# Down projections of an MoE kernel: each pass of a contraction chunk goes to both token tiles in turn

## What is computed

```python
for e in range(E):                       # 8 experts, D = 512, F = 1024
    mask = expert_idx == e
    h = np.maximum(x[mask] @ w1[e], 0.0)
    out[mask] = gate_w[mask, None] * (h @ w2[e])
...
h = np.maximum(x @ w_in, 0.0)            # 512 -> 2048
return (h * h @ w_out).astype(np.float32)    # 2048 -> 512
```

## Time and profile before

| what | value |
|---|---|
| median of 3 runs | 599.38 us |
| the three runs | 595.86, 599.38, 601.61 us |
| span of the profiled execution | 599.6 us |
| its mean granted TensorE clock | 0.980 |
| expert stage, first up matmul to the end of the last down | 139.0 to 307.6 us |
| feed-forward, first up matmul to the end | 319.1 to 599.6 us |

### The profile page before, as it was taken

The page is one execution under the profiler, slowest core; times in us unless marked ns, Lnnn a source line. Parts: engine busy times, 40 slices in busy tenths (PEclk is TensorE's granted clock), DMA queues, the critical chain, the costliest instruction groups (busy, mean ns, idle before and its releaser), DMA issues.

```text
span 599.6 us, 11061 instructions
## 1 busy us (share of the span) xinstructions
PE 578.1 (96%) x4259; PEld 506.3 (84%) x4259; DVE 285.5 (48%) x422; ACT 251.2 (42%) x517; POOL 95.7 (16%) x125
## 2 busy tenths in 40 slices
PE   7898999999999999999999999999999999999997
PEld 6776776599899898898888989889899998988986
DVE  5989886565556465475563223223323323222321
ACT  4788886824445544354452123222222212222221
POOL 7467850031022021130210000000000000000000
PEclk9789889989999999999999999999999999999999
DMA  7967896058676494684711002002001001000000
GB/s 223 262 201 209 227 188 181 27 176 303 233 272 224 149 317 134 226 281 147 271 62 44 1 1 72 0 1 70 0 0 70 0 0 69 1 0 36 1 0 36
DMA packets 66044, 70.68 MB, mean 118 GB/s; under 512 B 25784, under 2 KB 50360, under 8 KB 65632
## 3 DMA queue, kind: packets, MB, share of 16 engines
q1 hardware_dynamic: 62400, 58.17, 32.0%
q0 software_dynamic: 3616, 12.13, 5.8%
HBM read 60.22 MB, written 10.06 MB: 117 GB/s over the span
## 4 chain that ended last, share of the span: by engine, by line
PE 63%; issue 12%; DMA 11%; POOL 6%; DVE 4%; ACT 1%; SPq 1%; POOLq 1%; ACTq 0%; DVEq 0%
PE psum L799 19%; PE psum L801 19%; PE psum L800 19%; DMA x_rows_sb<-x_rows,idx_g 5%; DMA win_raw<-in_moe_w_in 3%; PE psum L592 3%; POOL win_lo L495 2%; DVE wa_lo L1340 2%; PE psum L793 1%; POOL win_hi L493 1%; DMA v_blk<-in_v 1%; ACT wa_hi L1019 1%; POOL v_blk L506 1%; PE psum L852 1%; DMA q_raw<-in_q 1%
## 5 line engine op out<-in xcount | busy, mean ns | idle before, releaser
L799 PE MATMUL psum<-x_hi,win_hi 128*128 128x256 f32 x384 | 108.4, 282 | 1.2 <-DVE x_lo L1388 1.2
L801 PE MATMUL psum<-x_hi,win_lo 128*128 128x256 f32 x384 | 108.4, 282 | 0.0
L800 PE MATMUL psum<-x_lo,win_hi 128*128 128x256 f32 x384 | 108.2, 282 | 0.0
L1398 DVE TENSOR_TENSOR h_sq<-h_relu 128x512 f32<-128x512 f32 x48 | 33.3, 694 | 133.4 <-ACT h_relu L1073 133.4
L1073 ACT ACTIVATE h_relu<-psum 128x512 f32<-128x512 f32 x48 | 28.7, 599 | 134.6 <-PE psum L801 134.6
L799 PE MATMUL psum<-wb_hi,h_hi 128*128 128x512 f32 x208 | 83.4, 401 | 0.0
L800 PE MATMUL psum<-wb_lo,h_hi 128*128 128x512 f32 x208 | 82.3, 396 | 0.0
L801 PE MATMUL psum<-wb_hi,h_lo 128*128 128x512 f32 x208 | 82.2, 395 | 0.0
L799 PEld LDWEIGHTS psum<-x_hi,win_hi 128*128 128x128 f32 x384 | 73.3, 191 | 2.9 <-issue 1.4
L800 PEld LDWEIGHTS psum<-x_lo,win_hi 128*128 128x128 f32 x384 | 73.3, 191 | 1.7
L801 PEld LDWEIGHTS psum<-x_hi,win_lo 128*128 128x128 f32 x384 | 73.3, 191 | 0.0
(11 more groups left out here) (184 smaller groups left out, 998.0 us busy)
## 6 DMA issues: line engine op xcount, KB each, us to landing
w_raw<-in_moe_w SPq DMA_DIRECT2D x56, 512.0 KB, 3.9
win_raw<-in_moe_w_in POOLq DMA_DIRECT2D x8, 512.0 KB, 5.8
w_raw<-in_moe_w_out SPq DMA_DIRECT2D x8, 512.0 KB, 4.0
k_raw<-in_k SPq DMA_DIRECT2D x8, 384.0 KB, 5.1
q_raw<-in_q SPq DMA_DIRECT2D x8, 384.0 KB, 5.0
v_blk<-in_v SPq DMA_DIRECT2D x3, 1024.0 KB, 6.0
v_win<-in_v SPq DMA_DIRECT2D x16, 192.0 KB
x_rows<-x_all SPq DMA_DIRECT2D x8, 384.0 KB, 4.7
```

What stands on the lines that cost most here:

```text
L799: pe.matmul(o, l_hi, r_hi, start=start, stop=False)
L800: pe.matmul(o, l_hi, r_lo, start=False, stop=False)
L801: return pe.matmul(o, l_lo, r_hi, start=False, stop=stop)
L1398: dve.tensor_tensor(h_sq[c % 2][:, :], h_relu[c % 2][:, :], h_relu[c % 2][:, :], ALU.mult)\
```

## The change

A new helper `three_both` issues the three passes of a product for both token tiles in turn: high by high for tile 0, then for tile 1, high by low for tile 0, then 1, low by high for tile 0, then 1. Successive matmuls so write the two banks of `ps_y` alternately, and the two of a pair have the same moving operand. In the feed-forward the sequence inside a chunk is all that changes. In `expert_down` the loop over token tiles goes inside the loop over chunks: both tiles are now summed over all 8 chunks together, both waits for the previous block's copies out of PSUM stand ahead, and `y_summed` gets its two increments from the last two matmuls of the whole down projection. What waits for `y_summed` on ACT and DVE is as it was. Thirteen empty lines at the top of the file also go, so that line numbers are 13 lower ahead of the new helper.

```diff
+            def three_both(l_hi, l_lo, r_hi, r_lo, start, stop):
+
+                for t in range(2):
+                    pe.matmul(ps_y[:, t, :], l_hi[t], r_hi, start=start, stop=False)
+                for t in range(2):
+                    pe.matmul(ps_y[:, t, :], l_hi[t], r_lo, start=False, stop=False)
+                return [pe.matmul(ps_y[:, t, :], l_lo[t], r_hi, start=False, stop=stop) for t in range(2)]
+
             def expert_down(b, first=False):
-                for t in range(2):
-                    if not first:
-                        pe.wait_ge(y_moved_dve if t else y_moved_act, b)
-                    for f in range(FC):
-                        if t == 0 and f % 2 == 0:
-                            pe.wait_ge(w_split[PIECES + f // 2], b + 1)
-                            pe.wait_ge(h_lo_made, 4 * b + f // 2 + 1)
-                        mm = three(ps_y[:, t, :], h_hi[:, f, t * P:(t + 1) * P], h_lo[:, f, t * P:(t + 1) * P],
-                                   wb_hi[:, f * DM:(f + 1) * DM], wb_lo[:, f * DM:(f + 1) * DM],
-                                   f == 0, f == FC - 1)
+                if not first:
+                    pe.wait_ge(y_moved_act, b)
+                    pe.wait_ge(y_moved_dve, b)
+                for f in range(FC):
+                    if f % 2 == 0:
+                        pe.wait_ge(w_split[PIECES + f // 2], b + 1)
+                        pe.wait_ge(h_lo_made, 4 * b + f // 2 + 1)
+                    both = three_both([h_hi[:, f, t * P:(t + 1) * P] for t in range(2)],
+                                      [h_lo[:, f, t * P:(t + 1) * P] for t in range(2)],
+                                      wb_hi[:, f * DM:(f + 1) * DM], wb_lo[:, f * DM:(f + 1) * DM],
+                                      f == 0, f == FC - 1)
+                for mm in both:
                     mm.then_inc(y_summed, 1)
...
                 for f in range(2):
                     at = (c % PIECES) * PIECE + f * DM
-                    for t in range(2):
-                        mm = three(ps_y[:, t, :], h2_hi[c % 3][:, f, t * P:(t + 1) * P],
-                                   h2_lo[c % 3][:, f, t * P:(t + 1) * P], hi[:, at:at + DM], lo[:, at:at + DM],
-                                   c == 0 and f == 0, c == PAIRS2 - 1 and f == 1)
+                    both = three_both([h2_hi[c % 3][:, f, t * P:(t + 1) * P] for t in range(2)],
+                                      [h2_lo[c % 3][:, f, t * P:(t + 1) * P] for t in range(2)],
+                                      hi[:, at:at + DM], lo[:, at:at + DM],
+                                      c == 0 and f == 0, c == PAIRS2 - 1 and f == 1)
                 if c == PAIRS2 - 1:
-                    mm.then_inc(y2_summed, 1)
+                    both[1].then_inc(y2_summed, 1)
```

## The result

The changed kernel took 642.92 us, the median of 4 runs (640.32 to 644.89), against 598.97 us for the kernel before. The ratio is 1.0711 with a 95% interval of 1.0665 to 1.0757: slower by 7%. The forecast was 640 us. The profiled execution took 643.24 us with a span of 641.5, 41.9 us more than the span of before, 599.6.

The account below looks back on a forecast made before the run. Bound by TensorE, 96% busy, and almost equally by the chain of waits through copies and gather in expert blocks. Terms 32.1 + 2.4 + 2.7 + 3.4 = 40.6 on 599.6 give 640.2, forecast 640 us, range 627 to 652.

Parts of the forecast that it names:

- The pace: 512-column matmuls in both stages: alternating banks changes their start-to-start distance by 0, bounds 2.7 us either way.
- the one rival on the other side: Second matmul of each down-projection pair gets cheap through its shared moving operand: 52.8 us less, 587.4 us; chance 0.04.
- One of the prediction's signs of being wrong: Feed-forward: the forecast counts as wrong if its length changes by over 2 us.
- Tile 0 is late: Expert blocks: ACT's tile 0 copy and the chain behind it shift 5.37 us per block, 32.1 us over six.
- The stall ahead of the up projection: PE stands idle about 2.9 us before each expert up projection, b = 1 to 6, until `wa_lo` is ready.
- chain and gather: Expert blocks: 32.1 us from the later chain plus 2.4 us from gathers meeting more weight loads.
- The second stall: PE waits about 3 us for the gather's DMA ahead of the transposes in each expert block.
- the first stall hides in the second: Expert blocks: the 2.9 us wait before the up projection isn't added; the period grows by 5.37 us in all.
- The end of the stage: End of the expert stage: DVE's last tile 1 copy shifts 3.7 us, 1.0 is spare, leaving 2.7 us.
- The clock: Low-clock stretches behind stalls in expert blocks and at feed-forward start: two of 1.7 us, 3.4 us; ends 0 and 11.9.
- The rival in which the clock falls nearly everywhere: Six expert blocks and the feed-forward start all pay for a low clock: 648.5 us; chance 0.12.
- the step from span to median: Whole kernel: the median of the runs was taken as 0.2 us below the profiled span.

Follow-up runs that it names:

- the kernel with the old sequence there: Kernel before with only the expert blocks' down projections alternating token tiles, feed-forward as before: 644.57 us, ratio 1.0745.
- with the second gone: Changed kernel with DVE's copy of tile 1 out of PSUM ahead of the four `wa_lo` pieces instead of behind them: 625.66 us, ratio 1.0414.
- The fillers: 22 filler transposes ahead of each expert up projection: on the changed kernel 655.48 us; on the changed kernel with DVE's tile 1 copy first 619.46 us.
- the kernel with the late increments: Kernel before, old matmul sequence, with only the two `y_summed` increments moved to the last two chunks of tile 1: 646.1 us, ratio 1.0657.

## Why the prediction was right, and where its sizes were off

*The pace.* Predicted 0 with bounds of 2.7 us. The feed-forward differs by 0.06 us over its 271.8, in the profile of the changed kernel, and the kernel with the change there alone has a ratio of 1.0005. The steps between banks that the kernel before already had in its trace had told as much. The 215.7 ns of the Trainium skill (TensorE: Matmul & The Clock Gate, "Wait — 56ns, not 53.3ns?") are not reached by alternating banks: the distance stayed at 233 ns, so whatever separates the two, it is not writes to the same bank. The shared moving operand gave nothing either, which removes the one rival on the other side.

One of the prediction's signs of being wrong did come true by the letter: the feed-forward changed by over 2 us, 282.7 for 280.5. All of the 2.2 us lie in its first stretch, at a clock of 0.78, and the kernel with the old sequence there has them too. The prediction had priced a low clock at just this place, and left it out of the sign.

*Tile 0 is late.* The copy was predicted at 0.03 us ahead of the end of the down projection, and is there (161.73, with the end at 161.76). The stall ahead of the up projection was predicted at 2.9 and is 2.73. The transposes were predicted at 17.5 to 18 us behind the end of a down projection; over the six blocks they come 17.0 to 19.2 behind it, 17.6 on average, where it was 12.0. So chain and gather together grew by 5.6 a block, 33.6 us in all, where 34.5 were predicted (32.1 + 2.4). The division was less good than the sum: the gather's DMA did not get slower (5.37 to 7.33 us, mean of five 6.0, before 5.99 to 6.80), and the extra lies ahead of it. In blocks 1, 3 and 5 the issue of the first gather DMA took 1.22 to 1.46 us instead of 0.99, and in blocks 4 and 6 POOL's copy of the indices took 0.91 us instead of 0.20. The second stall, predicted at about 3 us, was 0 to 4.6, and 1.8 on average, since the low clock made four up projections longer.

*That the first stall hides in the second* is borne out: with the second gone the time is 625.66 us, not that of before. The fillers say nothing on it, since they occupy the first stall without making it shorter; they show the same of the low clock behind it.

*The end of the stage.* Predicted 2.7, measured 3.9. DVE's copy came when expected, 3.8 us behind the end; the scatter behind it took 1.1 us longer from issue to the reading back of the rows (348.73 to 352.73, before 309.38 to 312.29), which had been taken as fixed.

*The clock.* Predicted 3.4 paid, two stretches of 1.7. Paid in the changed kernel: 1.6 in the down projection b = 4 (12.85 us for 11.28), 1.5 in transposes and down projection b = 6, and 2.2 at the start of the feed-forward, 5.3 in all. Two places in seven became three. The argument that a low stretch in the up projection makes one behind the second stall less likely was the right one: four of the six up projections were slow and hid it, the two that ran at full clock, b = 4 and 6, are the two in which it was paid (in the kernel with the late increments one block, b = 6, has both), and when the fillers took the slow ones away, the low clock moved to the paid side in every block. The rival in which the clock falls nearly everywhere was given 648.5 us; with the fillers, which bring it about, it is 655, since the low clock then cost 1.3 to 2.7 us a block, 2.0 on average, not 1.7, and the chain grew too.

That two places were taken was a choice between 0 and seven, not worked out; and that the errors of the terms go both ways and partly cancel is luck.

The sum of the smaller errors is +1.3 us (-0.9 chain, +1.2 end of the stage, +1.9 clock, -0.9 attention), which takes the 640.2 forecast for the span to the 641.5 measured. The remaining 1.6 us to the result (2.9 in all) are the step from span to median: the forecast took off 0.2 there, while the median lies 1.4 above the profiled span. What lies around the span had not been listed for the kernel before; in the changed kernel's profiled execution it is 1.7 (643.24 against 641.5). If it is as much in the kernel before, its profiled execution took about 601.3 us, 1.9 above the median, where the changed kernel's lies 0.3 above its own.

## What to carry to other kernels

A reordering inside one engine's work moves the moment at which each partial result is complete, and the time of a kernel can hang on that moment far more than on the pace: before interleaving two sums, look up who waits for the first one and what is queued behind that waiter. A trace that has both cases in it (here, steps that change the bank and steps that don't) answers the question of pace before anything is built. And when an engine waits twice per loop, price the waits together, with the clock: one may hide the other, and work put into the first can lengthen the second and cost more than it saves.

## What had not been expected

A low clock can be of use. In the changed kernel TensorE ran four up projections partly at its lower level, 13.2 us or more for 11.8, at next to no cost; with 2.4 us of filler in the first stall they ran at 1.00, and the kernel got 13 us slower, most of it because the second wait grew from 10.9 to 21.6 us over the stage and the lower level then fell into the transposes and down projections (clock 0.81 over the 14.7 us shown).

POOL's copy of the gather's indices, 0.2 us in the kernel before, took 0.91 in blocks 4 and 6 of the changed kernel and in all six with the fillers. Block 4 of the changed kernel, POOL and DVE:

```profile
258.15 0.91 POOL L539 COPY idx_g<-gather_tab 128x2 int32 x1
```

```profile
257.80 1.22 DVE L1337 TENSOR_TENSOR wb_lo<-w_raw,wb_hi 128x1024 fp32r<-128x1024 f32 x1
```

The copy starts while DVE makes a piece of `wb_lo` and ends at 259.06, 0.04 us behind it. In all twelve traces a copy that starts during such a subtraction ends 0.04 to 0.05 us behind it, and every other one takes 0.18 to 0.20. No run tests this by itself. In the changed kernel the two blocks are those whose up projection ran at full clock: there this `wb_lo` started 8.4 us behind the end of the down projection, in block 3, at the lower clock, 9.1. If the subtraction is what holds the copy up, a faster TensorE makes the gather later, and that would be a reason why the transposes come later with the fillers.

The change of bank has no price that these runs can see, in either direction: 0.2333 us within a bank, 0.2332 alternating, for 512 columns.
